# Routed experts after attention, one core: the seam between the two stages reordered (first expert tile, row table, paddings, zeroing)

## The reference, cut to what matters

```python
def sm_attn(qq, kk, vv): ...                 # softmax(scale * qq kk^T) vv
p_packed = sm_attn(p, k, v)                  # 32 packed rows for each of 8 x 8 heads
x = sm_attn(q, p_packed, p_packed)           # batch 8, heads 8, 576 tokens, 64 wide
x = x.transpose(0, 2, 1, 3).reshape(4608, 512)

xn, en = x / (norm(x) + 1e-6), expert_emb / (norm(expert_emb) + 1e-6)
logits = xn @ en.T / tau                     # 8 experts
expert_idx = argmax(logits, 1)
gate_w = softmax(logits)[arange(N), expert_idx]
for e in range(8):
    h = maximum(x[mask_e] @ w1[e], 0)        # 512 -> 1024
    out[mask_e] = gate_w[mask_e, None] * (h @ w2[e])

h = out @ w_in                               # 512 -> 2048
y = (h * sigmoid(h)) @ w_out                 # 2048 -> 512
```

## Time and profile before

| | us |
|---|---|
| median of 3 runs | 1462.63 (1462.43 to 1463.77) |
| the profiled execution, its own time | 1462.23 |
| its span, first to last instruction | 1460.4 |
| PE busy | 1414.0 (97%) |
| PEld busy | 1276.2 (87%) |
| DVE busy | 983.6 (67%) |
| POOL busy | 564.9 (39%) |
| ACT busy | 493.7 (34%) |

### The profile page before, as it was taken

One profiled execution on the slowest core, in us unless ns is written; L12 is line 12 of the kernel. 1 busy time (PEld: TensorE's weight loads), 2 busy tenths in 40 slices (PEclk: granted clock), 3 DMA queues, 4 the chain that ended last, 5 costly groups with the idle time before them and its releaser, 6 DMA issues. The chain is left out here.

```text
span 1460.4 us, 27820 instructions
## 1 busy us (share of the span) xinstructions
PE 1414.0 (97%) x9817; PEld 1276.2 (87%) x9818; DVE 983.6 (67%) x1380; ACT 493.7 (34%) x748; POOL 564.9 (39%) x466
## 2 busy tenths in 40 slices
PE   7999799999999999999999999999999999999996
PEld 4666588878888888888999999999989999999996
DVE  5887644444444444445888888888898778777783
ACT  4887400240001110203554354444463333333331
POOL 1566671597712771615653333333250111101111
PEclk9999999999999999999999999999999999999998
DMA  9994763476713552424344434444683343333430
GB/s 352 417 350 140 246 137 108 156 259 170 217 68 100 192 189 79 158 68 180 119 142 131 128 117 129 128 123 118 201 259 123 134 144 118 134 131 120 144 115 30
DMA packets 141768, 232.74 MB, mean 159 GB/s; under 512 B 11528, under 2 KB 94856, under 8 KB 134160
## 3 DMA queue, kind: packets, MB, share of 16 engines
q1 hardware_dynamic: 104128, 145.50, 30.4%
q10 hardware_dynamic: 26448, 58.12, 12.3%
q0 software_dynamic: 11136, 28.40, 5.8%
HBM read 144.86 MB, written 87.12 MB: 159 GB/s over the span
## 5 line engine op out<-in xcount | busy, mean ns | idle before, releaser
L785 PE MATMUL ps<-wf,xf 128*128 128x256 f32 x3024 | 365.1, 284 | 4.9 <-DVE xf L1830 4.1
L785 PEld LDWEIGHTS ps<-wf,xf 128*128 128x128 f32 x3024 | 364.5, 193 | 5.5 <-DVE xf L1830 2.8
L785 PE MATMUL ps<-xf,wf 128*128 128x256 f32 x2646 | 323.8, 284 | 0.1
L785 PEld LDWEIGHTS ps<-xf,wf 128*128 128x128 f32 x2646 | 319.1, 192 | 0.3 <-ACT cb L1250 0.3
L785 PE MATMUL ps<-weights,xT 128*128 (+1 forms) x1032 | 247.0, 394 | 4.1 <-DVE xT L1664 2.0
L785 PE MATMUL ps<-weights,hT 128*128 (+1 forms) x1032 | 246.6, 394 | 0.8 <-DVE hT L1716 0.8
L785 PEld LDWEIGHTS ps<-weights,xT 128*128 128x128 f32 x1032 | 190.5, 188 | 44.2 <-issue 6.1
L785 PEld LDWEIGHTS ps<-weights,hT 128*128 128x128 f32 x1032 | 190.6, 188 | 39.9 <-issue 1.1
L1972 POOL TENSOR_TENSOR weights<-stage,weights 128x1024 fp32r<-128x1024 f32 x56 | 132.5, 2412 | 159.7 <-ACT weights L1118 159.6
L1118 ACT CAST weights<-stage 128x1024 fp32r<-128x1024 f32 x56 | 57.9, 1051 | 396.2 <-PE ps L785 297.1
L2114 POOL TENSOR_TENSOR h<-h,sg 128x512 f32<-128x512 f32 x72 | 100.2, 1392 | 187.6 <-ACT sg L1264 187.4
(11 more groups left out here) (224 smaller groups left out, 1747.5 us busy)
## 6 DMA issues: line engine op xcount, KB each, us to landing
g_rows<-h SPq DMA_DIRECT2D x144, 256.0 KB, 2.6
raw<-g_rows SPq DMA_DIRECT2D x36, 1024.0 KB, 5.0
stage<-w ACTq DMA_DIRECT2D x53, 512.0 KB, 3.7
w_forms<-fm ACTq DMA_DIRECT2D x16, 896.0 KB
x_in<-x_rows SPq DMA_DIRECT2D x43, 256.0 KB
y_rows<-y_sb SPq DMA_DIRECT2D x43, 256.0 KB
wf_f<-w_forms SPq DMA_DIRECT2D x11, 896.0 KB, 5.4
q_sb<-qT SPq DMA_DIRECT2D x8, 1152.0 KB
```

Source lines behind the costliest of these rows:

```text
L785: mm = pe.matmul(o, left(a_), right(b_), start=first and n == 0, stop=last and n == 2)
```

## The change

The first tile's load waits for thresholds that now hold for both parities of batches, and the count behind them is taken over six batches instead of seven, inside the last batch (`first_count`). TensorE transposes the first tile right after the last ranks; ScalarE makes its high part and VectorE its low part ahead of the table's arithmetic. The table's matmuls stand inside the first up product (`up_first`), and the first down product comes right behind it, ahead of the second tile's up product; turn_x(1) stands in its middle. The second tile is loaded ahead of all pads. ScalarE no longer pads expert 0, SP does. Three blocks of rows (expert 0's first two tiles, expert 1's first) are zeroed early in the attention, and POOL's first scatter waits for that; the 2 MB of zeros goes out in front of the last batch. POOL's scatters of the last batch wait for the last ranks, and its low parts of expert 1's weights for the table. The last batch's ranks are in another bank. gates, places and keep_y(0) take other places in VectorE's order.

```diff
@@ -453,32 +459,30 @@
...
-            sp.sem_inc(pad0_out, 1)
+            sp.wait_ge(first_zero, 32)
             sp.wait_ge(need_done, 1)
-            enough_a = sp.value_load(need[0:1, 2:3], min_val=16 * EARLY_ROWS * (B // 2 - 1), max_val=16 * EARLY_ROWS * (B // 2))
-            enough_b = sp.value_load(need[0:1, 0:1], min_val=16 * LATE_ROWS * (B // 2 - 1), max_val=16 * LATE_ROWS * (B // 2))
-            padded = sp.value_load(need[0:1, 1:2], min_val=1, max_val=17)
-            sp.wait_ge(scat_a[0], 16 * EARLY_ROWS * (B // 2))
-            sp.wait_ge(scat_b[0], 16 * LATE_ROWS * (B // 2))
-            sp.wait_ge(scat_a[1], enough_a)
-            sp.wait_ge(scat_b[1], enough_b)
-            sp.wait_ge(pad0_out, padded)
+            enough_a = sp.value_load(need[0:1, 0:1], min_val=16 * EARLY_ROWS * (B // 2 - 1), max_val=16 * EARLY_ROWS * (B // 2))
+            enough_b = sp.value_load(need[0:1, 1:2], min_val=16 * LATE_ROWS * (B // 2 - 1), max_val=16 * LATE_ROWS * (B // 2))
+            for par in range(2):
+                sp.wait_ge(scat_a[par], enough_a)
+                sp.wait_ge(scat_b[par], enough_b)
             sp.dma_start(x_in, x_rows_d[0:P, :]).then_inc(x_in_done, 16)
...
             sp.wait_ge(tab_done, 1)
+            for par in range(2):
+                sp.wait_ge(scat_a[par], 16 * EARLY_ROWS * (B // 2))
+                sp.wait_ge(scat_b[par], 16 * LATE_ROWS * (B // 2))
+            load_x(1)
+            pad(2)
+            sp.wait_ge(x_in_done, 32)
+            pad(0)
             pad(1)
-            sp.wait_ge(scat_a[1], 16 * EARLY_ROWS * (B // 2))
-            sp.wait_ge(scat_b[1], 16 * LATE_ROWS * (B // 2))
-            sp.wait_ge(pad0_out, 17)
-            sp.wait_ge(pad_out, 16)
-            load_x(1)
-            for e in range(2, 4):
-                pad(e)
             sp.wait_ge(pad_out, 16 * 3)
             load_x(2)
+            pad(3)
             for e in range(4, E):
                 pad(e)
-            sp.wait_ge(pad_out, 16 * (E - 1))
+            sp.wait_ge(pad_out, 16 * E)
             sp.wait_ge(dummy_out, 16)
@@ -678,6 +682,9 @@
...
                     stay_warm(WARM, o=0 if last else 6)
+                if last:
+                    pe.wait_ge(acc_done, B - 2)
+                    pe.matmul(bank[1][0:1, 0:1], acc[:, 0:1], ones[:, 0:1], start=True, stop=True).then_inc(cnt0_done, 1)
                 if not first:
@@ -755,19 +760,6 @@
...
             ranks(B - 1, 1, SPLIT, TPB)
-            pe.wait_ge(acc_done, B)
-            pe.wait_ge(slot_done, B + 1)
-            pe.matmul(bank[2][0:E, 0:1], acc, ones[:, 0:1], start=True, stop=True)
-            pe.matmul(bank[3][0:1, T_PAD:T_PAD + E], ones[:, 0:1], acc, start=True, stop=True).then_inc(tab_step, 1)
-            pe.wait_ge(tab_step, 2)
-            pe.matmul(bank[2][0:E, 1:2], cs[0:E, C_INCL:C_INCL + E], cnt[:, 2:3], start=True, stop=True).then_inc(tab_step, 1)
-            pe.wait_ge(tab_step, 4)
-            for lhsT, r_, lo in ((cnt[:, 3:4], steps, T_ROW), (ones_f[0:E, :], steps, T_EXP),
-                                 (cnt[:, 2:3], cs[0:E, C_INCL:C_INCL + E], T_CUM)):
-                mm = pe.matmul(bank[3][0:1, lo:lo + r_.shape[1]], lhsT, r_, start=True, stop=True)
-            mm.then_inc(tab_step, 1)
@@ -828,25 +820,61 @@
...
                         pe.wait_ge(hT_lo, NT + 1)
+                    if isinstance(t, int) and t == 0 and c == KF // 2:
+                        turn_x(1)
                     if c % 2 == 0:
...
+            def counts():
+                pe.wait_ge(acc_done, B)
+                pe.wait_ge(slot_done, B + 1)
+                pe.matmul(bank[4][0:E, 0:1], acc, ones[:, 0:1], start=True, stop=True)
+                pe.matmul(bank[3][0:1, T_PAD:T_PAD + E], ones[:, 0:1], acc, start=True, stop=True).then_inc(tab_step, 1)
+            def tiles_before():
+                pe.wait_ge(tab_step, 2)
+                pe.matmul(bank[4][0:E, 1:2], cs[0:E, C_INCL:C_INCL + E], cnt[:, 2:3], start=True, stop=True).then_inc(tab_step, 1)
+            def table_rows():
+                pe.wait_ge(tab_step, 4)
+                for lhsT, r_, lo in ((cnt[:, 3:4], steps, T_ROW), (ones_f[0:E, :], steps, T_EXP),
+                                     (cnt[:, 2:3], cs[0:E, C_INCL:C_INCL + E], T_CUM)):
+                    mm = pe.matmul(bank[3][0:1, lo:lo + r_.shape[1]], lhsT, r_, start=True, stop=True)
+                mm.then_inc(tab_step, 1)
+            def up_first():
+                pe.wait_ge(xT_lo, 1)
+                pe.wait_ge(need_done, 1)
+                for c in range(KD):
+                    pe.wait_ge(w_done, c + 1)
+                    for n in range(2):
+                        lo = c * F + n * 512
+                        mm = three(bank[n], lambda a_: xT[:, a_, c, :], lambda b_: weights[:, 0, b_, lo:lo + 512],
+                                   c == 0, c == KD - 1)
+                        if c == 0:
+                            (table_rows if n else tiles_before)()
+                mm.then_inc(up_done, 1)
             pe.sem_inc(down_done, 1)
             turn_x(0)
+            counts()
             pe.wait_ge(w_done, KD)
-            stay_warm(2 * WARM, weights[:, 0, 0, 0:P], weights[:, 0, 0, 0:4 * P].rearrange("p (c k) -> p c k", c=4))
-            up(0, 0, True)
+            stay_warm(WARM, weights[:, 0, 0, 0:P], weights[:, 0, 0, 0:4 * P].rearrange("p (c k) -> p c k", c=4))
+            up_first()
             pe.wait_ge(gaps_done, 1)
...
             pe.wait_ge(tab_done, 1)
-            turn_x(1)
             turn_h(0)
+            down(0, 0, True)
             up(1, expert(1), False)
             turn_x(2)
-            down(0, 0, True)
             turn_h(1)
@@ -1080,8 +1108,9 @@
             act.wait_ge(zero_ready, 1)
-            act.dma_start(x_rows_d[DUMMY:NROW, :].rearrange("(o p) n -> p o n", p=P),
-                          zero.rearrange("p (o n) -> p o n", o=1).to_broadcast([P, E, DM])).then_inc(dummy_out, 16)
+            act.dma_start(x_rows_d[0:2 * P, :].rearrange("(o p) n -> p o n", p=P),
+                          zero.rearrange("p (o n) -> p o n", o=1).to_broadcast([P, 2, DM])).then_inc(first_zero, 16)
+            act.dma_start(x_rows_d[REG:REG + P, :], zero).then_inc(first_zero, 16)
             half = NROW // P
@@ -1092,21 +1121,22 @@
...
             batch(B - 2, B // 2 - 1, 0, more=False)
+            act.dma_start(x_rows_d[DUMMY:NROW, :].rearrange("(o p) n -> p o n", p=P),
+                          zero.rearrange("p (o n) -> p o n", o=1).to_broadcast([P, E, DM])).then_inc(dummy_out, 16)
             batch(B - 1, B // 2 - 1, 1, last=True)
-            for k in range(TPB):
+            keep_x(B - 1, B // 2 - 1, 1, 0, False)
+            for k in range(1, TPB):
                 keep_x(B - 1, B // 2 - 1, 1, k, False)
-            for k in range(TPB):
-                square_x(B - 1, 1, k)
+                square_x(B - 1, 1, k - 1)
+            act.wait_ge(xT_done, 1)
+            act.copy(xT[:, 0].rearrange("p c k -> p (c k)"), bank[2]).then_inc(xT_hi, 1)
+            square_x(B - 1, 1, TPB - 1)
...
             act.activation(st_all[:, 0, :], sq_all, ACT.Sqrt).then_inc(root_done, 1)
-            act.wait_ge(tab_done, 1)
-            row = act.value_load(table[0:1, T_PAD:T_PAD + 1], min_val=0, max_val=DUMMY - P)
-            act.dma_start(x_rows_d[bass.ds(row, P), :], zero).then_inc(pad0_out, 16)
@@ -1497,6 +1527,15 @@
...
                     dve.tensor_tensor(acc, acc, acc_add, ALU.add).then_inc(acc_done, 1)
+            def first_count():
+                dve.wait_ge(cnt0_done, 1)
+                dve.tensor_scalar(needf, bank[1][0:1, 0:1], float(P), -16.0, ALU.is_ge, ALU.mult).then_inc(need_part, 1)
+                dve.wait_ge(need_part, 1)
+                dve.tensor_scalar(need[:, 0:1], needf, float(EARLY_ROWS), 16.0 * EARLY_ROWS * (B // 2), ALU.mult, ALU.add)
+                dve.tensor_scalar(need[:, 1:2], needf, float(LATE_ROWS), 16.0 * LATE_ROWS * (B // 2), ALU.mult,
+                                  ALU.add).then_inc(need_done, 1)
@@ -1572,17 +1613,13 @@
...
             pick_experts(B - 1, 1, 7 * (B - 1), 0, SPLIT)
-            dve.wait_ge(cnt0_done, 1)
-            dve.tensor_scalar(needf, bank[1][0:1, 0:1], float(P), -16.0, ALU.is_ge, ALU.mult).then_inc(need_part, 1)
-            dve.wait_ge(need_part, 1)
-            dve.tensor_scalar(need[:, 0:1], needf, float(LATE_ROWS), 16.0 * LATE_ROWS * (B // 2), ALU.mult, ALU.add)
-            dve.tensor_scalar(need[:, 2:3], needf, float(EARLY_ROWS), 16.0 * EARLY_ROWS * (B // 2), ALU.mult, ALU.add)
-            dve.tensor_scalar(need[:, 1:2], needf, 17.0, None, ALU.add).then_inc(need_done, 1)
             make_slots(B - 1, 1, 7 * (B - 1) + 4, 0, SPLIT)
...
             make_slots(B - 1, 1, 7 * B + 4, SPLIT, TPB)
+            dve.wait_ge(xT_hi, 1)
+            dve.tensor_tensor(xT[:, 1].rearrange("p c k -> p (c k)"), bank[2], xT[:, 0].rearrange("p c k -> p (c k)").bitcast(F32),
```

(36 more changed lines are left out.)

15 lines of the change are left out of this document (9 added, 6 removed).

## The result

The changed kernel took 1473.78 us (median of 4 runs, 1472.13 to 1475.16) against 1462.62 of the kernel before beside it: ratio 1.0074, 95% interval 1.0057 to 1.0092. On another chip the same two gave 1473.14 and 1463.19: 1.0063, 1.0050 to 1.0075. So 9 to 11 us slower (the intervals reach from 7 to 13); forecast was 7.4. The profiled execution took 1474.61, its span is 1472.8. PE is busy 1418.9 us (before 1414.0), DVE 980.1 (983.6), POOL 564.8, ACT 493.4: the work is the same, TensorE waits more and runs more of it at half clock.

A forecast was written before the change was run, and what follows sets the result against it. TensorE, almost gapless in the tile loop, bounds the kernel, so the loop's start decides: 3.4 us later through the first up product, 2.3 for the order, 1.7 for the clock, sum 7.4: 1469.6 (median 1470.0), range 1466.0 to 1474.5.

The forecast's parts named there:

- The count: First tile's load: expert 0 has 0 tokens in six batches, so the test says no and all 40 scatters are awaited.
- rival 2: At the last ranks, VectorE's late release stays, 4.2 us more: sum 11.6, 1473.8 us. Chance 0.2.
- POOL's unbroken train: Eight scatters in a row held responsible for VectorE's 4.2 us wait for the last ranks; the new wait cuts the train.
- The stores: Last five scatters, their landing and the first load: x_in lands at 159.25, where before it was waiting in SBUF at 156.33.
- If that comes at 148.7, POOL starts at 148.9: Start of the last five scatters: with the last ranks done at 148.7, POOL begins them at 148.9.
- The first up product: Starts at 161.9, 2.4 us later; 5.62 plus 1.0 for the table's steps, ending at 168.5, 3.4 later.
- xT_lo at 161.75: First tile's low part ready at 161.75: load at 159.25, then transposes 1.11, ScalarE's copy about 0.6, VectorE's subtraction 0.69.
- Transposes 1.11 (at half clock, as before): First tile's transposes, after x_in lands at 159.25, take 1.11 us at half clock, as in the kernel before.
- the clock term: Behind the bare stretch before the first down product, one fall of 3.4 us at half speed: 1.7 us, bounds 0 and 3.4.
- The order of the products: First up product to the loop: first down product at once leaves ReLU, transposes and split bare; 20.5 against 18.2, 2.3 more.
- What costs nothing: Second tile's load, pads, x_in(3), POOL's low halves, 2 MB of zeros, early zero blocks, places and gates: covered, no cost.
- rival 3: No fall of the clock before the loop: sum 5.7, 1467.9 us. Chance 0.25.

The follow-up runs named there:

- both pairs: Two pairs of profiles, each the kernel before against the unaltered changed kernel: spans 1460.4 and 1472.8 us in the first, 1461.1 and 1470.3 in the repeat.
- experiment 9: Changed kernel with seven-batch count, old product order and 12 unread products before the first transposition: ratio 1.0010; then also without POOL's wait for the last ranks: 1.0010.
- experiment 2: Kernel before with only POOL's wait added, so the last batch's scatters wait for the last ranks: 1463.74 us, ratio 1.0024.
- experiment 8: Changed kernel with unread products in four gaps of TensorE and 48 more ahead of the first tile's transposition: 1469.96 us, ratio 1.0044.
- experiment 7: Changed kernel with unread products in four gaps of TensorE around the first two tiles' turned h: 1470.67 us, ratio 1.0045.
- experiments 1 and 3: Changed kernel with the count over seven batches again: 1466.52 us, ratio 1.0036; changed kernel without POOL's scatter wait: 1472.29 us, ratio 1.0079.
- experiment 10: First kernel of experiment 9, with ScalarE's first weight chunk held until the last row stores landed: 1466.16 us, ratio 1.0020.

## Why the forecast was right, and where it was short

The sign and the mechanism held; the sum of 7.4 stands against 10.0 and 10.1 us in the three stretches that both pairs share. The medians differ by 11.2 and 10.0.

- **The count.** Right: the test says no, the first load comes behind the last store (158.46 against 155.78), and going back to seven batches takes 4 to 5.5 us off the time (7.7 to 8.8 between the ranks and the third ReLU).
- **The late release (rival 2).** It went, as forecast, and with POOL's wait as the reason: the wait alone does it in the kernel before, where VectorE's instructions stay as they were, so that a fetch bound to their place in the code is no explanation. But "POOL's unbroken train" is not the whole condition: releases in the midst of a train were in time, the last ranks' once too, and the late ones end 0.1 us ahead of a store (experiment 9). The mechanism stays open. That it was priced as 4.2 us of gain was right only because of the first item: TensorE waits for the stores anyway. In the kernel before the same 4 us gain nothing (experiment 2).
- **The stores.** 2.9 forecast, 3.5 to 3.8 measured. The step "If that comes at 148.7, POOL starts at 148.9" is the short one: POOL's first store starts 1.0 us after the start of the ranks' last product, not 0.4. Pace (1.27), landing with the wait on SP (2.7) and the load (2.6) came as taken (1.26, 2.6 and 2.7).
- **The first up product.** 0.4 forecast from transposition to ReLU, 1.3 to 1.7 measured. The table inside was sized well: at full clock 6.6 us go from the product's start at 162.65 to ReLU at 169.26 (experiment 8), 5.62 and the 1.0 that was taken; from the transposition it is 8.7 us, where before 8.8 included 2.8 us at half. (In "xT_lo at 161.75" the terms given add up to 161.65.) The step that failed is "Transposes 1.11 (at half clock, as before)": I let the half clock end when it had ended before. With 11 us bare instead of 5, it lasts 13.7 us, to 166.1, and covers 5 us from the transposition on, 2.5 of them in the product. The bounds of the clock term held only the fall further on.
- **The order of the products.** 2.3 forecast; 2.5 at full clock (experiment 7).
- **The clock behind the bare stretch.** "One fall of 3.4 us", 1.7: of the changed kernel's two profiles one has one fall and one has two, 1.5 and 3.2 us; experiments 1 and 3, with the same order, have two. The second comes right at the loop's first product, after its gap of 1.07 and the one before it.
- **What costs nothing.** The pads, x_in(1), x_in(3), POOL's low parts, the 2 MB and the gates cost nothing: third to last ReLU take 494.8 and 494.3 against 495.0, and neither second nor fourth tile is waited for. This is read from the stretches behind the change; none of these parts was tried by itself.

The forecast's range, 1466.0 to 1474.5, held the time, and in part by luck: 1473.78 lies near the upper edge, which was drawn for the late release, and that did not happen. What brought the time there is the store term (0.6 to 0.9 us), the first up product (0.9 to 1.3), the second fall (1.5), and in the first pair 2.5 us of chance ahead of the ranks and at the end. The lower edge was set too low by its own terms: rival 3 with the table covered is 1462.23 + 5.7 - 1.0, which is 1466.9.

## What to carry to other kernels

A test that decides at run time has to be evaluated on the run's own data; here the eight choices of the reference decided the sign: read off the code alone, the change would have been forecast faster. Price a longer wait of TensorE twice, once as time and once as clock: how long the half clock lasts goes with how long the engine stood, and part of it falls on the work behind. Here 2.9 us bare went with 3.4 or 6.8 us at half, 5.3 to 5.4 with 6.8, and 9.4 to 11.4 with 10.2 or 13.7. And where two waits end close together, taking one away shows the other: find out what the next load waits for, and which transfers start in the same microsecond, before counting the gain.

## What was not expected of the hardware

**A fall of the clock costs by where it falls.** Twelve of the fourteen profiles have one between 1091 and 1115. Counted from the last ReLU, in six it begins after 406 to 408 us, and 776.2 to 776.4 us lie between that and the end, even where it lasts 6.8 us; in the other six it begins after 419.4 to 419.9, and that time is 777.5 to 777.7 with 3.4 us at half and 778.9 to 779.0 with 6.8. The two without it have 776.4. So the same fall costs nothing at one place and 1.2 us per 3.4 at the other, and two executions of the changed kernel differ in having it. The reason shows in TensorE's wait for VectorE's `xf`, which ends 420.1 to 420.4 us after the start of the last ReLU in all fourteen profiles. TensorE waits 2.9 us there in the eight without an early fall, 1.5 to 1.7 us in the five with one of 3.4 us, and 0.3 us in the one with 6.8. With no fall ahead of it (the changed kernel again), one of 3.4 us (the kernel before) and one of 6.8 (experiment 10):

```profile
1114.23 2.99 PE L777 MATMUL ps<-wf,xf 128*128 128x256 f32 x23 [2.95 <-DVE xf L1863]
```
```profile
1104.36 1.90 PE L785 MATMUL ps<-wf,xf 128*128 128x256 f32 x14 [1.51 <-DVE xf L1830]
```
```profile
1105.38 2.86 PE L777 MATMUL ps<-wf,xf 128*128 128x256 f32 x22 [0.27 <-DVE xf L1866]
```

The early fall makes TensorE's work longer inside a wait of 2.95 us and is paid from it. The later one (1115.0 in the changed kernel) lies across the end of that wait, and nothing takes up what comes after.

**VectorE behind POOL.** In experiment 2 two small operations (8 partitions by 8 elements) end only when three of POOL's products in a row are through:

```profile
155.56 7.55 DVE L1616 TENSOR_SCALAR gaps<-cs,cnt 8x8 f32<-8x8 f32 x1
155.69 7.42 DVE L1617 TENSOR_SCALAR gaps<-cs,cnt 8x8 f32<-8x8 f32 x1
...
156.00 13.99 POOL L1972 TENSOR_TENSOR weights<-stage,weights 128x1024 fp32r<-128x1024 f32 x6
161.64 1.48 DVE L1671 TENSOR_SCALAR h_sb<-ps 128x1024 f32<-128x1024 f32 x1
```

In the kernel before they took 0.21 us. They end at 163.1, and POOL's products run at about 2.36 us each from 156.00, so the third ends at 163.1. The Trainium skill ("SBUF — State Buffer", SBUF: two separate sides) calls the port pair that the two engines share an exclusive lock, held for a whole instruction. The row agrees in kind, but here VectorE was out for three instructions, not one. TensorE waited 1.57 us for the second of them (163.17, experiment 2), and the ReLU behind was 0.25 us longer. In this place it did no harm, since TensorE then waited 5.3 us more for the second tile anyway.
